# Experts of a mixture: tokens as the stationary operand for one-tile experts and third tiles

## What is computed

```python
def _moe2_ref(x, w_gate, w1, w2, capacity):      # x 1536 x 384, w1 8 x 384 x 1024, w2 8 x 1024 x 384
    logits = x @ w_gate
    expert_idx = np.argmax(logits, axis=1)
    ...                                           # gate_w: the softmax value of the chosen expert
    disp = np.zeros((E, capacity, D))             # the tokens of each expert in order, at most 384
    ...
    h = np.maximum(np.einsum('ecd,edf->ecf', disp, w1), 0.0)
    y = np.einsum('ecf,efd->ecd', h, w2)
    ...
    out[i] = gate_w[i] * y[expert_idx[i], pos[i]]
```

## Time and profile before

| | us |
|---|---|
| median of 3 runs | 448.55 |
| lowest and highest | 447.76, 449.93 |
| the profiled execution | 447.43 |
| its span, first to last instruction | 445.5 |
| TensorE busy in the span | 420.5 (94%) |
| VectorE, ScalarE, GpSimd busy | 257.6, 197.1, 176.3 |
| mean granted clock of TensorE | 0.991 |

### The profile page before, as it was taken

How to read it: one execution, slowest core, us unless ns; L and a number is a source line. 1 busy time by engine, 2 the same in 40 slices (tenths; PEclk the granted TensorE clock), 3 DMA queues, 4 the chain that set the end, 5 groups by cost and what they waited for, 6 DMA issues and landing times.

```text
span 445.5 us, 9385 instructions
## 1 busy us (share of the span) xinstructions
PE 420.5 (94%) x3333; PEld 406.7 (91%) x3333; DVE 257.6 (58%) x555; ACT 197.1 (44%) x450; POOL 176.3 (40%) x189
## 2 busy tenths in 40 slices
PE   5799999999999999999999986799999999998893
PEld 5688889999999999999999985699999999998893
DVE  6898867675435333643438564444668584648820
ACT  2799943432311123111223432244568674558731
POOL 3999725553323523244436860520110310012112
PEclk9999999999999999999999999999999999999997
DMA  7995034427960100000012440495676866563000
GB/s 248 403 355 188 3 113 147 151 89 253 371 220 14 40 1 0 0 23 31 0 35 71 142 147 15 141 346 191 185 235 190 258 193 204 159 214 107 10 19 7
DMA packets 33935, 61.45 MB, mean 138 GB/s; under 512 B 4654, under 2 KB 26910, under 8 KB 33888
## 3 DMA queue, kind: packets, MB, share of 16 engines
q1 hardware_dynamic: 31008, 55.53, 38.5%
q0 software_dynamic: 2880, 5.29, 3.5%
HBM read 47.53 MB, written 14.79 MB: 140 GB/s over the span
## 4 chain that ended last, share of the span: by engine, by line
PE 80%; DVE 7%; ACT 5%; issue 3%; POOL 2%; DMA 0%; POOLq 0%; DVEq 0%; ACTq 0%
PE bank L1152 20%; PE bank L1167 20%; PE bank L1277 17%; PE bank L1306 14%; ACT scores L613 3%; PE bank L1055 2%; PE bank L1264 1%; PE bank L1121 1%; ACT w_high L596 1%; DVE scores L828 1%; DVE neg L886 1%; PE bank L1085 1%; DVE act_full L892 1%; PE bank L1113 1%; PE bank L1176 1%
## 5 line engine op out<-in xcount | busy, mean ns | idle before, releaser
L512 POOL TENSOR_TENSOR g_low<-act_full,g_high 128x384 fp32r<-128x384 f32 x63 | 63.6, 1010 | 114.6 <-ACT g_high L642 114.6
L642 ACT ACTIVATE g_high<-act_full 128x384 fp32r<-128x384 f32 x64 | 33.7, 526 | 149.9 <-DVE act_full L892 137.3
L1152 PE MATMUL bank<-x_split,w_high 128*128 (+1 forms) x384 | 98.3, 337 | 0.0
L886 DVE TENSOR_SCALAR neg<-bank,alpha_sb 128x384 f32<-128x384 f32 x64 | 39.2, 613 | 71.5 <-PE bank L1152 71.4
L568 POOL DMA_INDIRECT out<-y_out,token x24 | 25.1, 1046 | 122.3 <-ACT y_out L729 121.0
L1152 PEld LDWEIGHTS bank<-x_split,w_high 128*128 128x128 f32 x384 | 69.0, 188 | 0.2 <-issue 0.2
L1167 PE MATMUL bank<-w_high,g_high 128*128 128x384 f32 x189 | 65.1, 344 | 1.1 <-POOL g_low L512 1.1
L1152 PE MATMUL bank<-x_split,w_low 128*128 (+1 forms) x192 | 64.4, 336 | 0.0
L1167 PE MATMUL bank<-w_high,g_low 128*128 128x384 f32 x189 | 63.8, 337 | 0.0
L1167 PE MATMUL bank<-w_low,g_high 128*128 128x384 f32 x189 | 63.7, 337 | 0.0
L1277 PE MATMUL bank<-xe_high,w_high 128*128 128x256 f32 (+1 forms) x192 | 58.0, 302 | 1.8 <-DVE xe_low L1005 1.8
(11 more groups left out here) (127 smaller groups left out, 794.2 us busy)
## 6 DMA issues: line engine op xcount, KB each, us to landing
w_raw<-chunks SPq DMA_DIRECT2D x96, 192.0 KB, 3.1
w_raw<-chunks SPq DMA_DIRECT2D x32, 384.0 KB, 3.2
rk_in<-att_rk SPq DMA_DIRECT2D x12, 704.0 KB, 6.1
routed_rows<-fill SPq DMA_DIRECT2D x1, 5211.0 KB, 16.8
xe<-routed_rows SPq DMA_DIRECT2D x7, 579.0 KB, 5.5
v_in<-att_v SPq DMA_DIRECT2D x12, 200.0 KB, 6.1
out<-fill SPq DMA_DIRECT2D x1, 2304.0 KB, 23.4
x_split<-x_split POOLq DMA_DIRECT2D x18, 48.0 KB, 2.7
```

What stands on the lines that cost most here:

```text
L512: pool.tensor_tensor(gl[:, f % 4, :], act_full[:, f % 2, :], gh[:, f % 4, :].bitcast(f32), ALU.subtract).then_inc(s_gl, 1)
L642: act.activation(gh[:, f % 4, :], act_full[:, f % 2, :], ACT.Copy).then_inc(s_gh, 1)
L886: dve.tensor_scalar(neg[:, f % 2, :], h, 0.0, alpha_sb[:, f:f + 1], ALU.min, ALU.mult)\
L1152: last = mm(bank[f % 4][:, 0:G], a[:, f, w], x[:, kc, bass.ds(g * G, G)], start=kc == 0 and i == 0, stop=kc == KC - 1 and i == 2)
```

## The change

It has five parts.

- A one-tile expert gets its own branch. Its tokens are the stationary operand and the weights move: `flip_up` makes half of the hidden layer (512 columns) with 9 products, tokens on the partitions. VectorE rectifies the result into a new tile `expert_g_by_token` (`flip_relu`), TensorE turns it back in four transposes of 128 (`flip_turn`), ScalarE copies the high part (`flip_high`) and VectorE subtracts (`flip_low`), each 512 wide. The next expert's three tiles of rows are turned between the two halves.
- A three-tile expert has its ups done 256 wide, then the third tile by the flipped form. The order of the down products is tile 1, 0, 2 there, and the output order everywhere 1, 2, 0. Tile 2 of the next rows is turned into bank 7.
- `flip_relu(e, 2)`, `flip_low(e, 2)` and `flip_high(e, 2)` are outside the branches: VectorE and ScalarE run them for each expert, also where there is no third tile. TensorE signals `s_fh[1]` and `s_ft[1]` for these.
- W1's low parts are made by GpSimd, ahead of the scatters of the expert in whose time they fall. W1's high parts wait for a signal (`s_w1free`) behind the ups and the third tile.
- Expert 0 starts with two tiles of rows; the third and the last three weight pieces follow within its ups. The rows of expert 1 are loaded ahead of the last two pieces.

The core of the diff (semaphores, bank waits and the parts for expert 0 left out):

```diff
-            for e in range(1, E):
-                for i in reversed(range(GT)):
-                    y_scatter(e - 1, i)
...
+            for e in range(E):
+                if e + FIRST < E:
+                    for f in range(NFE):
+                        split_low1(e + FIRST, f)
+                for i in Y_ORDER:
+                    y_scatter(e, i, s_out if e < E - 1 else s_last)
...
+            def flip_high(e, i, halves=(0, 1)):
+
+                act.wait_ge(s_step, e * NFE + FFN_STEPS)
+                act.wait_ge(s_yd[2], e)
+                for half in halves:
+                    act.wait_ge(s_ft[i // 2], 2 * e + half + 1)
+                    act.activation(egh[:, half * HF:(half + 1) * HF, i * P:(i + 1) * P],
+                                   bank[2 + half][:, :].rearrange("p (f n) -> p f n", f=HF), ACT.Copy)\
+                       .then_inc(s_fc[i // 2], 1)
...
+                flip_high(e, 2)
                 for f in range(NFE):
                     if e + FIRST < E:
                         split_high1(e + FIRST, f)
                     if f in (3, 5, 7):
-                        y_copy(e, (7 - f) // 2)
+                        y_copy(e, Y_ORDER[(f - 3) // 2])
...
+            def flip_relu(e, i, half):
+
+                dve.wait_ge(s_fh[i // 2], 2 * e + half + 1)
...
+                dve.tensor_scalar(gn[:, half * HF * P:(half + 1) * HF * P], bank[half][:, :], 0.0, None, ALU.max)\
+                   .then_inc(s_fr[i // 2], 1)
...
+                for kc in range(KC):
+                    for m, (x, w) in enumerate(((xeh, wh), (xeh, wl), (xel, wh))):
+                        last = mm(bank[half][:, :].rearrange("p (f n) -> p f n", f=HF),
+                                  x[:, e % 2, kc, i * P:(i + 1) * P], w[:, slot:slot + HF, kc * P:(kc + 1) * P],
+                                  start=kc == 0 and m == 0, stop=kc == KC - 1 and m == 2)
+                last.then_inc(s_fh[i // 2], 1)
...
             for e in range(E):
-                pe.wait_ge(s_tel, e * GT + GT)
+                with pe.If(rows[e] < P + 1):
+                    pe.wait_ge(s_tel, e * GT + GT - 1)
+                    pe.sem_inc(s_mh, NFE)
+                    for half in range(2):
+                        flip_up(e, 0, half)
...
+                    flip_turn(e, 0, (0,))
+                    if e < E - 1:
+                        for i in range(GT):
+                            if e:
+                                x_bank_free(e, i)
+                            turn_xe(e + 1, i, bank[X_BANK[i]])
+                    flip_turn(e, 0, (1,))
+                    no_tile(e, 1)
+                with pe.Else():
...
+                    expert_ups(e, 2 * P)
+                    expert_down(e, 1)
                 with pe.If(rows[e] < 2 * P + 1):
-                    expert_ups(e, 2 * P)
-                    turned(e, 2)
-                    pe.sem_inc(s_yd[2], 1)
+                    pe.sem_inc(s_w1free, 1)
+                    pe.sem_inc(s_fh[1], 2)
+                    no_tile(e, 2)
+                    expert_down(e, 0, range(HF + 1))
+
+                    pe.wait_ge(s_mgl, e * NFE + NFE + C_MGL)
+                    pe.sem_inc(s_ft[1], 2)
+                    expert_down(e, 0, range(HF + 1, NFE))
                 with pe.Else():
-                    expert_ups(e, CAP)
-                    expert_down(e, 2)
...
+                    for half in range(2):
+                        flip_up(e, 2, half)
+                    pe.sem_inc(s_w1free, 1)
+                    expert_down(e, 0, range(HF))
+                    flip_turn(e, 2)
+                    expert_down(e, 0, range(HF, NFE))
                     expert_down(e, 2)
```

More of the change, by code:

```diff
@@ L736, in _ @@
             split_high(2 * NF - 4)
[L737 removed]
+            for i in range(GT - 1):
                 xe_high(0, i, bank[4 + i])
[L739 to L747 removed]
@@ L749, in _ @@
-            for e in range(E):
-                with act.If(rows[e] < 2 * P + 1):
-                    ups(e, 2 * P)
-                with act.Else():
-                    ups(e, CAP)
+            def flip_high(e, i, halves=(0, 1)):
[6 more added lines that the diff above has]
+                       .then_inc(s_fc[i // 2], 1)
```

222 lines of the change are left out of this document (167 added, 55 removed).

## The result

| | before | change |
|---|---|---|
| median of four runs each, us | 448.15 | 454.35 |
| lowest and highest | 447.24, 449.93 | 453.44, 454.89 |
| ratio of the times, 95% interval | | 1.011 (1.009 to 1.014) |
| the profiled execution, its span | 447.43, 445.5 | 454.89, 452.9 |
| mean granted clock | 0.991 | 0.974 |

A forecast was written before the change was run, and what follows sets the result against it. TensorE was taken to bound experts 0 to 4, VectorE's low halves the changed experts 5 and 6. Terms -0.5 + 1.2 + 0.9 - 1.8 - 1.3 - 2.8 = -4.3 us gave 444.2 from 448.55; range 442.3 to 448.8.

The forecast's parts named there:

- 512 columns: Flipped up products on TensorE: 0.227 us each, continued from the 384-column pace, with bounds of 0.214 and 0.239.
- experts 0 and 4: Three-tile experts: narrower ups save 3.55 and 3.87 us, flipped ups and transposes back add 4.75; sum +1.2 and +0.9.
- experts 1 to 3: Two-tile experts: same products, W1's low splits on GpSimd and two idle ScalarE copies fit in; change 0.
- rival D: Up products of 512 columns run slowly because weights move in four blocks; 451 us in total; chance 0.06.
- rival C: TensorE's signal amid the down products comes only when they are done, delaying ScalarE; 7.2 us lost, 451.4; chance 0.08.
- The start: Ahead of expert 0: up products wait for two tiles of rows instead of three, -0.5 us.
- VectorE bounds the one-tile experts: Experts 5 and 6: ups shrink to 4.09 us, but VectorE's low halves then bound; -1.8 and -1.3 us.
- 8.3 + 0.5: Expert 5: second next tile split 8.3 us after the start, plus 0.5 for VectorE slowed by GpSimd.
- Contention: GpSimd working beside VectorE slows VectorE's operations: 0.5 us added in expert 5, 0.7 in expert 6.
- 8.7 with the waits and the branch: Expert 5: TensorE's down products start 8.7 us after the expert's start, the second next tile being split at 8.3.
- Rival B: Clock halves after pauses in experts 5 and 6, 1.7 us each: once 445.9, chance 0.24; twice 447.6, chance 0.09.
- The third is free at 5.5 where it can start at 5.65: 0: End of expert 7: the third scatter is not held up by earlier scatters, so nothing is lost behind the last product.

The follow-up runs named there:

- the third form: Kernel before with the next rows' third tile turned into bank 7, plus separate 128-column up products for one-tile experts: 463.55 us, ratio 1.034 to the kernel before.
- straight code: The change with TensorE's one-tile form for experts 5 to 7 written out without branches: 450.02 us, ratio 1.002 to the kernel before.
- no idle work: The change with ScalarE's and VectorE's third-tile work skipped by a branch where there is no third tile: 451.80 us, ratio 1.008 to the kernel before.
- W1's splits on VectorE: The change with W1's low parts made by VectorE again and GpSimd only scattering: 451.62 us, ratio 1.006 to the kernel before.
- all repairs: The change with one branch per one-tile expert, idle third-tile copies left out, VectorE's W2 splits after the low parts: 449.20 us, ratio 1.000 to the kernel before.
- one branch: The change with a one-tile expert's ups, signals and down products in one TensorE branch instead of two: 451.51 us, ratio 1.007 to the kernel before.
- straight code with the splits last: The change with branch-free TensorE code for experts 5 to 7, idle third-tile work skipped, W2 splits behind the next rows: 446.36 us, ratio 0.994 to the kernel before.

## Why the prediction was wrong

- **512 columns, experts 0 and 4, experts 1 to 3.** The price of 0.227 (measured 0.229) and the signs held; both three-tile experts came 0.2 dearer, the cost of the transposes back (0.9 instead of 0.66: the 0.083 each left out the slower restart that the prediction names itself). Products of 512 columns at 0.229 refute rival D, ScalarE's idle copies at 13.3 refute rival C in experts 1 to 3.
- **The start.** The -0.5 held: TensorE's wait ahead of expert 0 fell from 1.77 to 1.41, and from the first transpose of its rows to its first up product it takes 2.4 instead of 3.0. But these transposes begin at 286.05 in the one profile and at 287.19 in the other, and where they begin varies between executions of kernels that are alike up to there (286.05 to 288.40 with three tiles of rows, 285.84 to 287.42 with two). So does the start of expert 0: 288.2 to 289.8 with two tiles, 289.06 to 291.40 with three (the third form, with its 7.96, left out). Some 1.1 us of the miss are this spread.
- **VectorE bounds the one-tile experts.** Right, and well sized: the second next tile was split 9.05 after expert 5's start, against 8.3 + 0.5. Contention was taken as 0.5 and 0.7; removing it was worth 0.7 and 1.0.
- **The step that failed first: "8.7 with the waits and the branch".** I allowed 0.4 from the split to the down products, and nothing later. It took 1.3, and the code behind the branch came late once more, by 1.2 in expert 6 and 0.85 in expert 7. In straight code 0.75 to 0.79 are left of the 1.3: some 0.5 is the jump, and 0.35 more than I allowed stands between the wait and the product without one. The evidence that I used, a seamless start in expert 7 of before, came from a TensorE that had products queued up to there; the pauses that I forecast myself take that backlog away. The Trainium skill, "Runtime: NRT & Kernel Launch", section "Instruction fetch mechanics", says that instructions arrive in blocks of 16 KiB and that a taken branch out of the loaded pages has to fetch its target first. The packets agree with it. I had not weighed this rule.
- **Rival B, which the sum put at nothing.** The forecast took both pauses at full clock, and this is the largest term that it lacked: 4.2 us. The mechanism and its size of 1.7 were right for expert 5 (down products 5.84 instead of 4.29), in expert 6 it took 2.6 as the stall prolonged it. But the case that happened, both pauses, had a chance of 0.09; the change and four variants (no idle work, W1's splits on VectorE, straight code, all repairs) had it twice, two (one branch, straight code with the splits last) once, and with the jumps gone and the pauses filled it did not happen.
- **"The third is free at 5.5 where it can start at 5.65: 0".** The margin of 0.15 went with the late sequencer: the signal stands behind the same code, and the end grew by 1.4. That is rival C's mechanism after all, in expert 7 alone: it had the output copies start 3.6 behind the start of the down products and 1.9 lost at the end; they started 4.0 behind it (443.00) and 1.4 were lost.

Summed over the profiled executions, the miss of 11.7 us is: slow clock 1.6 + 2.6, 0.9 + 0.6 + 0.5 ahead of the down products, late code 1.2 + 0.85 within them, the end 1.4, the start 1.1, experts 0 and 4 0.5: 11.3. Another 0.25 is VectorE in expert 5, the rest rounding. Of the first two of the three terms ahead of the down products some 0.5 each is the jump. The third, expert 7's, is no matter of code: D is 6.34 there in the change and in straight code alike, where 5.8 was forecast. The transposes back and the hand-overs between the engines were priced too low (0.72 from the first of them to ScalarE's copy, where 0.35 and a share of 0.1 stood).

What stays open is why of two like pauses one lowered the clock and the other not, and what the 0.75 between the last wait and the first down product are made of.

## What to carry to other kernels

A pause in TensorE's queue has three prices, of which only the first is seen in the old profile: the pause itself, the slow clock behind it, and the loading of code behind the next jump, which a backlog had hidden. Before fewer products are bought with such a pause, ask who bounds that stretch; here it was VectorE, and a freed PSUM bank gave 2.9 us where the change as a whole lost 6. The new form won in the same experts only when the branches were gone and the splits moved out of its way. Work put on GpSimd isn't free for VectorE where both subtract tiles in SBUF.

## What the hardware showed that I had not expected

- Jumps cost TensorE 0.5 to 2.2 us, and 6.7 ahead of expert 0 with three forms in the code. Code added elsewhere moved the places: with 24 transposes more in experts 5 and 6, expert 7 had no late product.
- With a new stationary block for each, a product of 128 columns takes 0.112 us, of 256 0.120, of 384 0.173, of 512 0.229: below 256 columns nothing is to be had.
- VectorE's subtraction of two SBUF tiles goes from 0.54 to between 1.0 and 1.23 beside GpSimd's, while that from PSUM stays at 0.41.
- The clock fell after a pause with TensorE busy 1.28 of 4 us, and after a like one it did not.
